# Gated linear attention before two mixtures of experts: the recurrence in chunks of 64 tokens in place of 128, and the last expert weighed in its hidden blocks

## The chip, the cores and the metric

The kernel is one program on one core of a Trainium2 chip. A core has five engines, each with its own queue of instructions: TensorE (PE in the rows, its weight loads PEld), VectorE (DVE), ScalarE (ACT), GpSimd (POOL) and SyncE (SP), which here only starts DMAs. They wait for each other through semaphores. PE multiplies a stationary block held in a 128x128 array by a moving block and writes to eight PSUM banks of 128 partitions by 512 floats. The metric is the device time of one execution in microseconds, median of several.

## The reference

For 4 sequences of 768 tokens and 8 heads with 48 channels, a gated recurrence gives `y`; two feed-forward stages follow on all 3072 tokens.

```
state = alpha[t, :, None] * state + k[t] (x) v[t]      # per head, 48 x 48
y[t]  = q[t] @ state
h = x @ w_in                       # 384 -> 2048
g = h if h > 0 else exp(h) - 1
x2 = g @ w_out                     # 2048 -> 384
p = domain_probs / (sum(domain_probs) + 1e-9)
out = sum over 4 experts e of p[:, e] * (relu(x2 @ w1[e]) @ w2[e])   # 384 -> 1024 -> 384
```

## The kernel before, in words

**The feed-forward work** runs in 6 tiles of 512 tokens. A tile has 48 steps: 16 of the first stage (ELU) and 8 for each of 4 experts (ReLU). In step J of a tile PE computes the hidden block of step J+2 into `ps_h` (`hidden`, 9 matmuls of 512 columns), and then adds the block of step J into three banks `ps_o` (`output`, 9 matmuls). The 9 are 3 blocks times 3 products: each operand is split in a high and a low fp32r part, and high x low, low x high and high x high are added (L568 to L570). ACT makes the high part and DVE the low part, of each weight block (L927, L744), of each hidden block (L953 or L958, then L761 or L765), of the input `x` and of `x2`. PE waits before `output(J)` for `g_ready`, and before `hidden(n)` for the bank of block n-2 and the weights. In the last step of the ELU stage (J = 15) there is no `hidden` ahead: PE does `output(15)` and then `first_experts`, which needs `x2`, split by ACT and DVE from the banks that `output(15)` has just filled.

**The attention** runs in 12 units of 256 tokens. Two are done ahead of the first tile (functions with "early" in the name). The other ten, u = 2 to 11, are cut in pieces and dealt out between the steps: table `PARTS_AT` gives a step at which each kind of work starts, and a unit's "piece" i comes i steps later. In PE's queue a piece stands between `hidden(J+2)` and `output(J)`; in step 15 it stands between `output(15)` and `first_experts`. Even units from u = 4 start in step 5 of a tile, odd ones in step 28; units 2 and 3 start in steps 15 and 28 of tile 0. DVE, ACT and POOL take the events of step J-1 in their step J.

A chunk of 128 tokens is halved again and again: level l couples right and left spans of 2^l tokens. Levels 0 to 3 are done on DVE and POOL in blocks of 16 tokens, whose scores go out to memory and come back as `pair_weights`. Levels 4, 5 and 6 are matmuls of q and k (L440), whose results ACT copies as rectangles into `pair_weights` (L876), while DVE and POOL carry the decays into q (L730) and k (L1083). Then PE transposes the keys (L495), forms the outer products of keys and values (`outer`, L513, 32 columns of the array, 48 moving columns), DVE adds them to a state that POOL has decayed (L739, L1095), and `attend` gives the outputs of each chunk: 28 matmuls of a 128x32 stationary tile by 128 moving columns (L537 from the state, L541 and L546 from `pair_weights`). Four such tiles, side by side in the array's columns, run at once. Heads go in pairs: one head's 48 channels in partitions 0 to 47, the other's in 64 to 111.

The pieces of a unit are: level 4 at i = 0, level 5 at 2, level 6 at 4, keys at 6, outer products at 8, outputs of both chunks at 10. They share three PSUM banks `ps_att` in turn. PE sees one fp32 matmul as two records; an fp32r matmul is one.

**The end.** After the last block DVE multiplies each of three banks by the last expert's weight into `part` (L791), POOL adds it to `acc` (L1103), and SP stores `acc` (L376). There are two `part` buffers.

Of the kernel before, what the change touches and what calls it, by code (L numbers as in the profile page):

```python
# [5 lines left out]
F32 = mybir.dt.float32  # L6
# [12 lines left out]
LEVELS = 7  # L19
# [6 lines left out]
UNIT = 2 * P  # L26
UNITS = TOKENS // UNIT
# [16 lines left out]
BANK_AT = {("L", LOW): 0, ("L", LOW + 1): 2, ("L", LOW + 2): 4, ("K", 0): 6, ("KV", 0): 8, ("Y", 0): 9}  # L44
NBANK = 11
# [58 lines left out]
for lag in range(LEVELS - 2):  # L104
    EARLY_ORDER += [(0, lag + 2), (1, lag)]
EARLY_ORDER += [(1, LEVELS - 2), (1, LEVELS - 1)]

# [11 lines left out]
COUNTS = {"low": LEVELS, "block": PARTS + 1, "piece": max(PIECES) + 2}  # L119
# [9 lines left out]
def is_elu(n):  # L129
    return n % STEPS < N1  # L130

# [12 lines left out]
def program(nc, q_d, k_d, a_d, v_d, qb_d, kb_d, ab_d, k0_d, v0_d, w_d, probs_d, eye_d, masks_d, sc_d, pn_d, out):  # L144
    ctx = ExitStack()
    with ctx:
# [15 lines left out]
        TD += [sbs(f"decay{1 << l}", 2, [P, PAIRS, UNIT >> l]) for l in range(1, LEVELS + 1)]  # L162
        VT = sbs("v_tok", 2, [P, 2, PAIRS, P])
        PW = sb("pair_weights", [P, 2, HEADS, P])
        KS = sbs("k_tok", 2, [P, PAIRS, P])
        ST = sbs("state", 3, [P, PAIRS, 2 * D])
# [12 lines left out]
        ex = sbs("elu_exp", 2, [P, TILE])  # L179
        gt = sbs("elu_out", 2, [P, TILE])  # L180
# [7 lines left out]
        v0 = part[1][0:1, 0:PAIRS * 2 * D].rearrange("p (a e) -> p a e", a=PAIRS)  # L188
        early_w = pb[:].rearrange("p e t -> p (e t)").rearrange("p (c a t) -> p c a t", c=2, a=HEADS)
        weights = [PW[:], early_w]  # L190
# [36 lines left out]
        p_step = sem("p_step")  # L227
# [22 lines left out]

        def y_bank(g):
# [4 lines left out]
        def queries(g):  # L256

            return chunk(QT, g)

        def pair_weights(g):  # L260
            return weights[g // 2 if g < EARLY else 0][:, g % 2]
# [32 lines left out]
        def rectangles(banks, w, l, sd):  # L294

            h = 1 << l
            dst = w.rearrange("p c (a s) t -> p s c a t", s=2)[:, sd]
            if l < LEVELS - 1:
                src = banks[sd][:, 0:2 * PAIRS * h].rearrange("p (c a t) -> p c a t", c=2, a=PAIRS)
                for m in range(HALF // h):  # L300
                    rows = slice(2 * m * h, (2 * m + 1) * h)
                    yield dst[rows, :, :, (2 * m + 1) * h:(2 * m + 2) * h], src[rows]
            else:
                src = banks[sd][:, 0:PAIRS * h].rearrange("p (c a t) -> p c a t", c=2, a=PAIRS // 2)
                for i in range(2):
                    yield dst[0:h, :, 2 * i:2 * i + 2, h:2 * h], src[h * i:h * (i + 1)]

        @block.sync
        def _(sp):
# [39 lines left out]
            def place_scores(u):  # L349
# [4 lines left out]
                for c in range(2):  # L354
                    for b in range(P // SUB):
                        rows = slice(SUB * b, SUB * (b + 1))
                        sp.dma_start(PW[rows, c, :, rows], sc_d[u].rearrange("(h b) (s t) -> b s h t", h=HEADS, t=SUB)[P // SUB * c + b]
                                     ).then_inc(pw_in, 16)
# [55 lines left out]
        def _(pe):  # L414
            def bank_free(u, i):
# [8 lines left out]
                elif i == BANK_AT["KV", 0]:  # L424
                    pe.wait_ge(st_ready, 2 * u + 3)
                else:
                    pe.wait_ge(xa_ready, 2 * u + i - BANK_AT["Y", 0] + 1 - EARLY)

            def level(banks, s, l):

                h = 1 << l
                for c in range(2):
                    if l < LEVELS - 1:
                        blocks_of = [(pr, m, 2 * m * h, (PAIRS * c + pr) * h) for pr in range(PAIRS) for m in range(HALF // h)]
                    else:
                        blocks_of = [(2 * i + b, 0, i * h, (PAIRS // 2 * c + b) * h) for b in range(PAIRS // 2) for i in range(2)]
                    for pr, m, row, col in blocks_of:
                        for sd in range(2):
                            r, first = slice(HALF * sd, HALF * (sd + 1)), P * c + 2 * m * h
                            last = nc.tensor.matmul(banks[sd][row:row + h, col:col + h], KL[s][r, pr, first:first + h],  # L440
                                                    QT[s][r, pr, first + h:first + 2 * h], start=True, stop=True)
# [11 lines left out]
            def early_pairs(u, l):  # L453
# [12 lines left out]
                if l == LEVELS - 1:  # L466
                    level(banks, u, l).then_inc(e_step[u], 1)
                    return
# [11 lines left out]
            def first_state():  # L480
                pe.wait_ge(first_in, 32)
                for pr in range(PAIRS):
                    last = nc.tensor.matmul(ps_l[1][1][0][:, pr * 2 * D:(pr + 1) * 2 * D], k0[:, pr, :], v0[:, pr, :], start=True, stop=True)
                last.then_inc(kv_done, 1)

            def transpose_k(g):
                if g < EARLY:
                    pe.wait_ge(e_k[g // 2], LEVELS)
                    pe.wait_ge(e_rect[g // 2], LEVELS - 1 - MASKED)
# [8 lines left out]

            def outer(u):
                if u < LEAD:  # L500
                    pe.wait_ge(e_rect[u], LEVELS - MASKED)
                else:
                    bank_free(u, BANK_AT["KV", 0])
                o, s = kv_bank(u), u % 2
                pe.wait_ge(v_in[s], 16 * (u // 2 + 1))
                for c in range(2):
                    pe.wait_ge(ks_ready, 2 * u + c + 1)
                    for pr in range(PAIRS):
                        col = (PAIRS * c + pr) * D
                        for i in range(P // COL):  # L510
                            rows = slice(COL * i, COL * (i + 1))
# [4 lines left out]
            def attend(g):  # L516
                s = g // 2 % 2
                if g < EARLY:
                    pe.wait_ge(e_near, g // 2 + 1)
                    pe.wait_ge(e_rect[g // 2], LEVELS - MASKED)  # L520
                    pe.wait_ge(e_q[g // 2], LEVELS)
                    pe.wait_ge(ks_ready, min(g + 1, EARLY - 1))
                else:
                    pe.wait_ge(pw_in, 16 * 2 * (P // SUB) * (g // 2 - LEAD + 1))
                    pe.wait_ge(rect, 2 * lev(g // 2, LEVELS - 1))
                    pe.wait_ge(q_up, lev(g // 2, LEVELS - 1))
                    bank_free(g // 2, BANK_AT["Y", 0] + g % 2)
                o = y_bank(g)
                pe.wait_ge(st_ready, g + 1)
                pe.wait_ge(v_in[s], 16 * (g // 4 + 1))  # L530
                v = VT[s][:, g % 2]
                for kt in range(KT):
                    dst = [o[COL * i:COL * (i + 1), kt * P:(kt + 1) * P] for i in range(P // COL)]
                    heads = [4 * kt + i if kt < KT - 1 else 2 * i for i in range(P // COL)]
                    for d, head in zip(dst, heads):
                        left = D - COL // 2 if kt == KT - 1 else head % 2 * 2 * COL
                        nc.tensor.matmul(d, ST[g % 3][:, head // 2, left:left + COL], queries(g)[:, head // 2, :], start=True, stop=False)  # L537
# [649 lines left out]
```

## Time and profile before

| | |
|---|---|
| median of 3 runs | 1324.49 us (1324.25 to 1326.15) |
| profiled execution, its own time | 1323.65 us |
| its span, first to last instruction | 1321.6 us |
| granted TensorE clock, mean | 0.999 |
| busy: PE, DVE, ACT, POOL | 98%, 64%, 46%, 41% |

The span is what the rows cover; 2.05 us of the execution's own time lie outside it. "Busy" of PE counts the time in which at least one matmul is under way, and a matmul's own time (0.39 us for 512 columns) overlaps the next: what one costs is the distance from start to start. In a timeline row the columns are the start in us from the span's beginning, the time until the last of the merged instructions ends, engine, line, operation, tiles, shapes and the number of instructions.

### The profile page before, as it was taken

The numbers are of one execution on the slowest core, as the hardware profiler recorded it, in microseconds if no ns is written. First come the engines' busy times: TensorE is split into PE (matmuls) and PEld (weight loads), VectorE is DVE, ScalarE is ACT, GpSimd is POOL, SyncE is SP. The second block draws the span as 40 slices with busy tenths as digits, with TensorE's granted clock in tenths as the row PEclk, the third lists the DMA queues.
The fourth block names the chain that finished last, engine by engine and source line by source line (L and its number), as shares of the span: only waits on it lengthen the run. The fifth ranks groups of instructions, "written<-read, shape, count | busy, mean of one in ns | idle before, by whom it ended". The sixth has DMA issues, their size and how long they took to land.

```text
span 1321.6 us, 26257 instructions
## 1 busy us (share of the span) xinstructions
PE 1299.6 (98%) x10472; PEld 1070.5 (81%) x10472; DVE 844.8 (64%) x1121; ACT 607.1 (46%) x1051; POOL 537.6 (41%) x457
## 2 busy tenths in 40 slices
PE   6899999999999999999999999999999999999998
PEld 6787888888888888888888888888888888888886
DVE  7786767765676765576776567666557645654443
ACT  3656343367434347534336733435653433653331
POOL 1671948611755831453851175682155311100012
PEclk9999999999999999999999999999999999999999
DMA  5545263255244236235335524423633233523330
GB/s 199 179 132 174 80 198 90 87 171 169 87 150 147 75 102 215 98 108 201 89 99 170 170 85 144 144 86 110 203 103 113 86 98 86 155 90 108 96 96 24
DMA packets 84028, 165.77 MB, mean 125 GB/s; under 512 B 30146, under 2 KB 31683, under 8 KB 83908
## 3 DMA queue, kind: packets, MB, share of 16 engines
q1 hardware_dynamic: 83616, 163.97, 40.0%
q8 instruction: 83, 1.36, 0.4%
q14 instruction: 37, 0.30, 0.1%
q10 hardware_dynamic: 292, 0.13, 0.0%
HBM read 157.99 MB, written 6.08 MB: 124 GB/s over the span
## 4 chain that ended last, share of the span: by engine, by line
PE 88%; issue 5%; DVE 4%; ACT 2%; POOL 1%; DMA 0%; POOLq 0%; ACTq 0%; DVEq 0%
PE ps_o L568 14%; PE ps_h L568 13%; PE ps_h L569 13%; PE ps_h L570 13%; PE ps_o L569 13%; PE ps_o L570 13%; PE ps_att L440 2%; DVE w_lo L744 1%; PE ps_att L537 1%; PE ps_att L513 1%; POOL acc L1103 1%; DVE elu_out L757 1%; PE ps_att L495 1%; PE ps_att L541 1%; PE ps_att L546 1%
## 5 line engine op out<-in xcount | busy, mean ns | idle before, releaser
L744 DVE TENSOR_TENSOR w_lo<-w_stage,w_hi 128x768 fp32r<-128x768 f32 x288 | 341.5, 1186 | 30.7 <-ACT w_hi L927 27.1
L958 ACT ACTIVATE g_hi<-ps_h 128x512 fp32r<-128x512 f32 x192 | 114.8, 598 | 499.9 <-PE ps_h L570 499.8
L568 PE MATMUL ps_o<-g_hi,w_lo 128*128 128x512 f32 x864 | 342.5, 396 | 0.6 <-DVE g_lo L761 0.6
L568 PE MATMUL ps_h<-x_hi,w_lo 128*128 128x512 f32 x864 | 337.8, 391 | 2.7 <-DVE x_lo L751 1.3
L569 PE MATMUL ps_o<-g_lo,w_hi 128*128 128x512 f32 x864 | 336.7, 390 | 0.0
L570 PE MATMUL ps_o<-g_hi,w_hi 128*128 128x512 f32 x864 | 336.7, 390 | 0.0
L569 PE MATMUL ps_h<-x_lo,w_hi 128*128 128x512 f32 x864 | 336.3, 389 | 0.0
L570 PE MATMUL ps_h<-x_hi,w_hi 128*128 128x512 f32 x864 | 336.3, 389 | 0.0
L765 DVE SCALAR_TENSOR_TENSOR g_lo<-ps_h,g_hi 128x512 fp32r<-128x512 f32 x192 | 132.3, 689 | 262.4 <-ACT g_hi L958 262.1
L927 ACT CAST w_hi<-w_stage 128x768 fp32r<-128x768 f32 x288 | 239.4, 832 | 13.7 <-DMA w_stage<-in_w 12.7
L275 POOL TENSOR_TENSOR products<-blocks 128x384 f32<-128x384 f32 x150 | 195.3, 1316 | 87.1 <-DVE scores L680 81.5
L1103 POOL TENSOR_TENSOR acc<-acc,part 128x512 f32<-128x512 f32 x54 | 77.1, 1456 | 315.3 <-DVE part L791 315.3
L568 PEld LDWEIGHTS ps_h<-x_hi,w_lo 128*128 128x128 f32 x864 | 162.1, 188 | 40.7 <-issue 4.2
L568 PEld LDWEIGHTS ps_o<-g_hi,w_lo 128*128 128x128 f32 x864 | 162.1, 188 | 36.5 <-issue 1.2
L570 PEld LDWEIGHTS ps_o<-g_hi,w_hi 128*128 128x128 f32 x864 | 162.2, 188 | 34.3
L570 PEld LDWEIGHTS ps_h<-x_hi,w_hi 128*128 128x128 f32 x864 | 162.2, 188 | 33.9
L569 PEld LDWEIGHTS ps_h<-x_lo,w_hi 128*128 128x128 f32 x864 | 162.2, 188 | 33.4
L569 PEld LDWEIGHTS ps_o<-g_lo,w_hi 128*128 128x128 f32 x864 | 162.3, 188 | 31.9
L1083 POOL TENSOR_TENSOR k_level<-k_level,decay 128x512 f32<-128x512 f32 x30 | 36.2, 1206 | 230.9 <-PE ps_att L440 230.9
L761 DVE TENSOR_TENSOR g_lo<-elu_out,g_hi 128x512 fp32r<-128x512 f32 x96 | 70.8, 739 | 61.1 <-ACT g_hi L953 61.1
L757 DVE SCALAR_TENSOR_TENSOR elu_out<-elu_exp,ps_h 128x512 f32<-128x512 f32 x96 | 65.8, 685 | 65.1 <-ACT elu_exp L947 65.1
L953 ACT CAST g_hi<-elu_out 128x512 fp32r<-128x512 f32 x96 | 59.6, 621 | 94.1 <-DVE elu_out L757 60.2
(100 smaller groups left out, 999.1 us busy)
## 6 DMA issues: line engine op xcount, KB each, us to landing
w_stage<-in_w SPq DMA_DIRECT2D x288, 384.0 KB, 3.1
k_level<-in_k SPq DMA_DIRECT2D x12, 512.0 KB, 5.6
q_low<-in_q SPq DMA_DIRECT2D x12, 512.0 KB, 6.4
alpha<-in_a SPq DMA_DIRECT2D x12, 512.0 KB, 4.1
v_tok<-in_v SPq DMA_DIRECT2D x12, 512.0 KB, 5.1
p_rows<-p_norm SPq DMA_DIRECT2D x6, 1024.0 KB, 9.0
out<-acc SPq DMA_DIRECT2D x18, 256.0 KB, 3.9
blocks<-in_q_blocks SPq DMA_DIRECT2D x10, 384.0 KB, 4.0
```

The lines of the kernel that those rows point to most:

```text
L275: return engine.tensor_tensor(dst, q[:, :, 1, i:i + 1, :].broadcast_to([P, pairs, h, D]), k[:, :, 0], ALU.mult)
L568: nc.tensor.matmul(dst, lhs[1], rhs[0], start=first, stop=False)
L569: nc.tensor.matmul(dst, lhs[0], rhs[1], start=False, stop=False)
L570: return nc.tensor.matmul(dst, lhs[0], rhs[0], start=False, stop=last)
L744: nc.vector.tensor_tensor(wl[n % WRING][:], stage[n % STAGE][:], wh[n % WRING][:].bitcast(F32), ALU.subtract).then_inc(w_low, 1)
L757: nc.vector.scalar_tensor_tensor(gt[n % 2][:], ex[n % 2][:], -1.0, ps_h[n % 2][:], ALU.add, ALU.max).then_inc(h_read, 1)
L761: nc.vector.tensor_tensor(gl[n % GS][:], gt[n % 2][:], gh[n % GS][:].bitcast(F32), ALU.subtract).then_inc(g_ready, 1)
L765: nc.vector.scalar_tensor_tensor(gl[n % GS][:], ps_h[n % 2][:], 0.0, gh[n % GS][:].bitcast(F32), ALU.max, ALU.subtract).then_inc(g_ready, 1)
L927: nc.scalar.copy(wh[n % WRING][:], stage[n % STAGE][:]).then_inc(w_hi, 1)
L953: nc.scalar.copy(gh[n % GS][:], gt[n % 2][:]).then_inc(g_hi, 1)
L958: nc.scalar.activation(gh[n % GS][:], ps_h[n % 2][:], ACT.Relu).then_inc(g_hi, 1)
L1103: nc.gpsimd.tensor_tensor(acc[:, m, :], acc[:, m, :], part[k % 2][:], ALU.add).then_inc(acc_added, 1)
```

## The change

In the ten later units the recurrence goes in spans of 64 tokens. Level 6 is gone (`LEVELS` 7 to 6). The outer products are made for each span of 64 tokens: the same number of matmuls, but with 64 rows, 64 columns of the array and 64 moving columns, into two banks, one for each side. There are four new states in a unit instead of two, in a layout of 64 columns in which the head pair lies on row halves. DVE makes each with four instructions that multiply, add and read PSUM at once; POOL's decay (L1095) is gone there. The outputs are 128 matmuls of a 64x32 stationary tile by 64 moving columns, in two pieces: 64 from `pair_weights` and 32 from the states at i = 9, and the other 32 from the states, with row halves exchanged, at i = 11. The early units keep chunks of 128; their states lie in `acc` and one array of pair weights in the ELU buffers, and the state tiles there are 64 instead of 48 columns wide in PSUM. Last, for the final 8 blocks of all (the last expert of the last tile), DVE multiplies the hidden block by the expert's weight before it is split, and the end is an addition of PSUM to `acc` on DVE alone.

```diff
-LEVELS = 7
+EARLY_LEVELS = 7
+LEVELS = 6
+SPANS = UNIT // HALF
-CLEARS = 5
+CLEARS = 6
-PIECES = {0: ("L", LOW), 2: ("L", LOW + 1), 4: ("L", LOW + 2), 6: ("K", 0), 8: ("KV", 0), 10: ("Y", 0)}
-NBANK = 11
+PIECES = {0: ("L", LOW), 2: ("L", LOW + 1), 4: ("K", 0), 6: ("KV", 0), 9: ("Y", 0), 11: ("Y", 1)}
+NBANK = 10
+STATES_AT = {6: (0,), 7: (1, 2), 8: (3,)}
+X_AT = {11: 0, 12: 1}
...
+def is_weighed(n):
+    return n >= ALL - NE
...
-                    nc.tensor.matmul(ps_l[1][1][0][:, pr * 2 * D:(pr + 1) * 2 * D], k0[:, pr, :], v0[:, pr, :], start=True, stop=True)
+                    nc.tensor.matmul(ps_l[1][1][0][:, pr * P:(pr + 1) * P], k0[:, pr, :], v0[:, pr, :], start=True, stop=True)
...
             def outer(u):
...
-                            v = VT[s][:, c, pr, i // 2 * HALF:i // 2 * HALF + D]
-                            last = nc.tensor.matmul(o[rows, col:col + D], KS[c][:, pr, rows], v, start=True, stop=True)
+                        for i in range(2):
+                            for side in range(2):
+                                r, rows = slice(HALF * side, HALF * (side + 1)), slice(HALF * i, HALF * (i + 1))
+                                last = nc.tensor.matmul(kv_banks(u)[side][rows, col:col + HALF], KS[c][r, pr, rows], VT[s][r, c, pr, rows],
+                                                        start=True, stop=True)
...
+            def state_part(u, turn):
+                for c in range(2):
+                    for wide in range(2):
+                        for pr in range(PAIRS):
+                            for span in range(2):
+                                sd = span ^ turn
+                                r, first, left = slice(HALF * sd, HALF * (sd + 1)), P * c + HALF * span, COL * (sd ^ wide)
+                                last = nc.tensor.matmul(y_part(u, c, span, KT - 1 if wide else sd, pr),
+                                                        ST[(SPANS * (u - LEAD) + 2 * c + span) % STATES][r, pr, left:left + COL],
+                                                        QT[u % 2][r, pr, first:first + HALF], start=False, stop=(turn == c == wide == 1))
+                return last
+
+            def value_part(u):
+                for c in range(2):
+                    for sd in range(2):
+                        for wide in range(2):
+                            for pr in range(PAIRS):
+                                for span in range(2):
+                                    r, left = slice(HALF * span, HALF * (span + 1)), HALF * sd + COL * (sd ^ wide)
+                                    nc.tensor.matmul(y_part(u, c, span, KT - 1 if wide else sd, pr), VT[u % 2][r, c, pr, left:left + COL],
+                                                     PW[r, c, 2 * pr + sd, :], start=(c == sd == wide == 0), stop=False)
+
+            def attend(u):
...
+                value_part(u)
+                pe.wait_ge(st_ready, states_before(u, SPANS - 1))
+                state_part(u, 0).then_inc(y_done, 1)
+
+            def attend_other(u):
+                pe.wait_ge(y_done, 2 * u + 1)
+                state_part(u, 1).then_inc(y_done, 1)
...
+            def state(u, k):
...
+                for pr in range(PAIRS):
+                    col = (PAIRS * (k // 2) + pr) * HALF
+                    last = nc.vector.scalar_tensor_tensor(ST[(g + 1) % STATES][:, pr, :], ST[g % STATES][:, pr, :], TD[LEVELS][u % 2][:, pr, k:k + 1],
+                                                          kv_banks(u)[k % 2][:, col:col + HALF], ALU.mult, ALU.add)
...
+            def weigh_hidden(n):
+                dve.wait_ge(h_full, n + 1)
+                nc.vector.scalar_tensor_tensor(gt[n % 2][:], ps_h[n % 2][:], 0.0, pb[:, EXPERTS - 1, :], ALU.max, ALU.mult).then_inc(weighed, 1)
+                lower_elu(n)
+
+            def add_last(t):
...
+                    nc.vector.tensor_tensor(acc[:, m, :], ps_o[m][:], acc[:, m, :], ALU.add).then_inc(acc_added, 1)
...
-            weigh(TILES - 1, EXPERTS - 1)
+            add_last(TILES - 1)
```

How instructions move, at two places. First PE's queue in tile 1, around steps 14 to 16, where the outputs of unit 4 stand. Before, in step 15, after the last product of `output(15)` and ahead of `first_experts`:

```order
L570 MATMUL ps_o<-g_hi,w_hi 128x512
L537 MATMUL ps_att<-q_low,state 32x128 x4
L541 MATMUL ps_att<-pair_weights,v_tok 32x128 x4
L537 MATMUL ps_att<-q_low,state 32x128 x4
L541 MATMUL ps_att<-pair_weights,v_tok 32x128 x4
L537 MATMUL ps_att<-q_low,state 32x128 x4
L546 MATMUL ps_att<-pair_weights,v_tok 32x128 x8
...
L568 MATMUL ps_h<-x_hi,w_lo 128x512
```

(the middle six rows come once more, for the second chunk). Now, in step 14 between `output(13)` and `output(14)`, and the rest in step 16 between `hidden(18)` and `output(16)`:

```order
L659 MATMUL ps_o<-g_hi,w_hi 128x512
L616 MATMUL ps_att<-pair_weights,v_tok 32x64 x64
L602 MATMUL ps_att<-q_low,state 32x64 x32
L657 MATMUL ps_o<-g_hi,w_lo 128x512
...
L659 MATMUL ps_h<-x_hi,w_hi 128x512
L602 MATMUL ps_att<-q_low,state 32x64 x32
L657 MATMUL ps_o<-g_hi,w_lo 128x512
```

The 56 matmuls have become 96 and 32, and no piece stands in step 15 of tiles 1 to 4 any more.

Second, DVE's queue where an odd unit's states are made, among weight splits (`w_lo`) and hidden splits (`g_lo`). Before (L739 is the addition to the state):

```order
L739 TENSOR_TENSOR state<-ps_att,state 64x4x48 [waits state_decayed,kv_done]
L739 TENSOR_TENSOR state<-ps_att,state 64x4x48
L680 TENSOR_REDUCE scores<-products 128x2x4 [waits product] x2
L744 TENSOR_TENSOR w_lo<-w_stage,w_hi 128x768 [waits w_hi_ready]
L765 SCALAR_TENSOR_TENSOR g_lo<-ps_h,g_hi 128x512 [waits g_hi_ready]
```

Now, in the step with two states:

```order
L840 SCALAR_TENSOR_TENSOR state<-state,decay_1,ps_att 128x64 [waits decay_ready,y_done,kv_done,state_ready]
L840 SCALAR_TENSOR_TENSOR state<-state,decay_1,ps_att 128x64 x3
L840 SCALAR_TENSOR_TENSOR state<-state,decay_1,ps_att 128x64 [waits decay_ready,y_done,kv_done,state_ready]
L840 SCALAR_TENSOR_TENSOR state<-state,decay_1,ps_att 128x64 x3
L758 TENSOR_TENSOR q_low<-q_low,decay_0 128x128x4 [waits decay_ready,q_low_updated]
L846 TENSOR_TENSOR w_lo<-w_stage,w_hi 128x768 [waits w_hi_ready]
L866 SCALAR_TENSOR_TENSOR g_lo<-ps_h,g_hi 128x512 [waits g_hi_ready]
```

Eight short instructions stand ahead of the splits in that step, and four in the step before and in the one after it; before there were two in each of two steps.

## Rows read from the trace of the kernel before

**Rows 1.** The profile's page: PE's busy time, and the chain that ended last.
```profile
PE 1299.6 (98%) x10472; PEld 1070.5 (81%) x10472; DVE 844.8 (64%) x1121; ACT 607.1 (46%) x1051; POOL 537.6 (41%) x457
PE 88%; issue 5%; DVE 4%; ACT 2%; POOL 1%; DMA 0%; POOLq 0%; ACTq 0%; DVEq 0%
```
**Rows 2.** PE's waits: line, who ended them, us in total, times, longest.
```profile
PE ps_o L483 <- DMA part<-in_v_first: 4.5, 1, 4.5
PE ps_h L568 <- DVE x_lo L751: 1.3, 1, 1.3
```
**Rows 3.** Timeline of PE, tile 1, around level 5: eight matmuls, piece, nine matmuls.
```profile
299.80 0.39 PE L568 MATMUL ps_h<-x_hi,w_lo 128*128 128x512 f32 x1
...
301.61 0.39 PE L570 MATMUL ps_h<-x_hi,w_hi 128*128 128x512 f32 x1
301.93 0.76 PE L440 MATMUL ps_att<-q_low,k_level 64*32 64x32 f32 x64
...
304.81 0.39 PE L568 MATMUL ps_h<-x_hi,w_lo 128*128 128x512 f32 x1
```
**Rows 4.** The same around level 4.
```profile
292.05 0.39 PE L570 MATMUL ps_h<-x_hi,w_hi 128*128 128x512 f32 x1
292.37 1.22 PE L440 MATMUL ps_att<-q_low,k_level 64*16 64x16 f32 x128
...
295.71 0.39 PE L568 MATMUL ps_h<-x_hi,w_lo 128*128 128x512 f32 x1
```
**Rows 5.** The same around level 6.
```profile
310.70 0.39 PE L570 MATMUL ps_h<-x_hi,w_hi 128*128 128x512 f32 x1
311.02 0.69 PE L440 MATMUL ps_att<-q_low,k_level 64*64 64x64 f32 x32
...
313.82 0.39 PE L568 MATMUL ps_h<-x_hi,w_lo 128*128 128x512 f32 x1
```
**Rows 6.** The same around the outer products.
```profile
328.78 0.39 PE L570 MATMUL ps_h<-x_hi,w_hi 128*128 128x512 f32 x1
329.10 0.89 PE L513 MATMUL ps_att<-v_tok,k_tok 128*32 128x48 f32 x64
...
332.08 0.39 PE L568 MATMUL ps_o<-g_hi,w_lo 128*128 128x512 f32 x1
```
**Rows 7.** The same around the outputs of unit 5 (112 records in between).
```profile
440.76 0.39 PE L570 MATMUL ps_h<-x_hi,w_hi 128*128 128x512 f32 x1
...
446.47 0.40 PE L568 MATMUL ps_h<-x_hi,w_lo 128*128 128x512 f32 x1
```
**Rows 8.** Timeline, tile 5, steps 14 to 15, where no attention is left.
```profile
1181.26 0.69 DVE L761 TENSOR_TENSOR g_lo<-elu_out,g_hi 128x512 fp32r<-128x512 f32 x1 [0.69 <-ACT g_hi L953]
1182.47 0.39 PE L568 MATMUL ps_o<-g_hi,w_lo 128*128 128x512 f32 x1
1184.28 0.39 PE L570 MATMUL ps_o<-g_hi,w_hi 128*128 128x512 f32 x1
1184.86 0.47 PE L568 MATMUL ps_h<-x_hi,w_lo 128*128 128x512 f32 x1 [0.19 <-DVE x_lo L771]
```
**Rows 9.** Timeline of the end: PE's last matmul, POOL's and DVE's last work.
```profile
1315.62 0.39 PE L570 MATMUL ps_o<-g_hi,w_hi 128*128 128x512 f32 x1
1315.46 3.71 POOL L1103 TENSOR_TENSOR acc<-acc,part 128x512 f32<-128x512 f32 x3 [23.49 <-DVE part L791]
1316.84 0.69 DVE L791 TENSOR_TENSOR part<-ps_o,p_rows 128x512 f32<-128x512 f32 x1 [0.78 <-POOL acc L1103]
```
**Rows 10.** Groups by line: busy us, mean ns of one, idle before.
```profile
L739 DVE TENSOR_TENSOR state<-ps_att,state 64x192 f32<-64x192 f32 x48 | 16.8, 351 | 0.9 <-PE ps_att L513 0.5
L765 DVE SCALAR_TENSOR_TENSOR g_lo<-ps_h,g_hi 128x512 fp32r<-128x512 f32 x192 | 132.3, 689 | 262.4 <-ACT g_hi L958 262.1
L797 DVE TENSOR_SCALAR p_sum<-p_sum 128x24 f32<-128x24 f32 x1 | 0.6, 644 | 0.0
```
**Rows 11.** Timeline of DVE before step 0.
```profile
54.62 0.69 DVE L757 SCALAR_TENSOR_TENSOR elu_out<-elu_exp,ps_h 128x512 f32<-128x512 f32 x1
```

More of the change, by code:

```diff
@@ L118, with states_before @@
 }
-COUNTS = {"low": LEVELS, "block": PARTS + 1, "piece": max(PIECES) + 2}
+COUNTS = {"low": LEVELS, "block": PARTS + 1, "piece": max(X_AT) + 1}
+def states_before(u, k):
+    return EARLY + 1 + SPANS * (u - LEAD) + k
 def segment(n):
@@ L249, in kv_bank, with kv_banks @@
             return ps_l[0][u][1 - u] if u < LEAD else bank_of("KV", u, 0)
+        def kv_banks(u):
+            return [bank_of("KV", u, side) for side in range(2)]
         def y_bank(g):
@@ L497, in transpose_k, with early_outer @@
                 last.then_inc(kt_done, 1)
-            def outer(u):
[L500 to L504, printed above, removed]
+            def early_outer(u):
+                pe.wait_ge(e_rect[u], EARLY_LEVELS - MASKED)
+                o = kv_bank(u)
+                pe.wait_ge(v_in[u], 16)
+                for c in range(2):
+                    pe.wait_ge(ks_ready, 2 * u + c + 1)
+                    for pr in range(PAIRS):
+                        col = (PAIRS * c + pr) * HALF
+                        for i in range(P // COL):
+                            rows = slice(COL * i, COL * (i + 1))
+                            v = VT[u][:, c, pr, i // 2 * HALF:(i // 2 + 1) * HALF]
+                            last = nc.tensor.matmul(o[rows, col:col + HALF], KS[c][:, pr, rows], v, start=True, stop=True)
+                    last.then_inc(kv_done, 1)
+            def outer(u):
+                s = u % 2
+                for side in range(2):
+                    bank_free(u, BANK_AT["KV", 0] + side)
                 pe.wait_ge(v_in[s], 16 * (u // 2 + 1))
@@ L548, in attend @@
-                last.then_inc(y_done, 1)
+                    dst = [o[COL * i:COL * (i + 1), kt * P:(kt + 1) * P] for i in range(PAIRS)]
+                    left = (0, HALF, COL)[kt]
+                    for pr, d in enumerate(dst):
+                        nc.tensor.matmul(d, early_st[g % 3][:, pr, left:left + COL], q[:, pr, :], start=True, stop=False)
+                    sides = (0, 1) if kt == KT - 1 else (kt,)
+                    for sd in sides:
+                        left = HALF * sd + COL * ((kt == KT - 1) != (sd == 1))
+                        for pr, d in enumerate(dst):
+                            last = nc.tensor.matmul(d, v[:, pr, left:left + COL], w[:, 2 * pr + sd, :], start=False, stop=(sd == sides[-1]))
@@ L562, in attention @@
                     outer(u)
-                else:
-                    for c in range(2):
-                        attend(2 * u + c)
+                elif l == 0:
+                    attend(u)
+                else:
+                    attend_other(u)
             def products(dst, lhs, rhs, first, last):
```

319 lines of the change are left out of this document (167 added, 152 removed).

## The prediction

> **What bounds the kernel now.** I read the page first: PE is busy 98% of the span, and the chain of work that ended last is PE for 88% [rows 1]. Then the list of PE's waits: apart from 4.5 us for the first DMA, the largest at the hidden blocks is 1.3 us, once [rows 2]. So PE's queue is full from the first hidden block to the last output, and the time is what PE's instructions cost from start to start, plus a head of about 50 us and a tail. Third, the timeline of PE around each kind of piece. Eight steps from one 512-column matmul to the next take 301.61 - 299.80 = 1.81 us, so 0.2265 us each [rows 3]. 5184 of them are 1174 us; that part is untouched. Between the last product of a hidden block and the first of the next lie ten such steps, 2.27 us; with a piece in between, what is above 2.27 is the whole price of the piece:
> level 4: 3.66 - 2.27 = 1.39 [rows 4]; level 5: 3.20 - 2.27 = 0.93 [rows 3]; level 6: 3.12 - 2.27 = 0.85 [rows 5]; outer products: 3.30 - 2.27 = 1.03 (nine matmuls and the step over the piece, again ten) [rows 6]; outputs: 5.71 - 2.27 = 3.44 [rows 7].
>
> **How these prices are made.** An fp32 matmul is two records. In level 6, 32 records in 0.69 us, of which the last alone is about 0.22: 0.47 us for 8 groups of four tiles, 59 ns a group [rows 5]. [...] Level 4 does not follow this: 128 records in 1.22 - 0.17 us are 8.2 ns a record, however few its columns are (16); that is the pace at which records can be started [rows 4]. What is left of each price is fixed, the change of tile shape and back: 0.85 - 0.47 = 0.38 in level 6, 1.03 - 0.68 = 0.35 in the outer products, 1.39 - 1.05 = 0.34 in level 4, and 3.44 - 28 x 0.109 = 0.39 in the outputs. I take 0.38.
>
> **The change, part by part, for each of the ten later units.**
> Level 6 goes: -0.85. With it go an update of q on DVE and of k on POOL and four copies on ACT; none of these held PE, so they count nothing.
> Outer products: 64 records in 16 groups of 2x2 tiles with 64 columns, the shape of level 6: 16 x 0.059 + 0.38 = 1.32, +0.29.
> Outputs: 128 matmuls are 256 records, in two pieces. Eight tiles (64x32) can be under way together. A group of eight would need 59 ns by columns, but 8 x 8.2 = 66 ns by the pace of starting, so the second decides: 192 x 0.0082 + 0.38 = 1.95, and 64 x 0.0082 + 0.38 = 0.90. Together 2.85, -0.59. No row shows eight tiles with so many columns at once. From below the price is 32 groups x 0.059 + 0.76 = 2.65; from above, if only four tiles run at a time, 64 x 0.059 + 0.76 = 4.54. I take 2.85, since rows 5 and 6 show both halves of the arrangement, and level 4, which uses the same eight places, kept its 8.2 ns.
> [...]
> Sum for a unit -0.85 + 0.29 - 0.59 = -1.15, for ten -11.5 us.
>
> **Step 15 of tiles 1 to 4.** Before, the outputs of the even unit stood between `output(15)` and the first expert and covered the splitting of x2 by ACT and DVE. Now nothing stands there. Tile 5 has no piece in that place either and shows the price: 1184.86 - 1184.28 = 0.58 instead of 0.23, and the first block after it is a little slow [rows 8]. 0.4 us, four times: +1.6. Below it is 0 (nothing else can gain), above perhaps 1.0 each if DVE comes late.
> Would it? In tile 5 the last split of block 15 ends at 1181.95, and `output(15)` starts at 1182.47: 0.5 us to spare [rows 8]. The new kernel puts eight state instructions ahead of it on DVE in step 13, but also 1.95 us of output piece on PE in step 14: 2.45 to spare. The size of a state instruction (128x64, reading PSUM): 192 columns take 351 ns, 512 take 689 [rows 10], so 1.06 ns a column and 148 fixed, 216 ns for 64 columns; eight are 1.7 us. Before there was nothing of this kind in that step. Part of it fills time in which DVE waited for ACT: it idles 262 us before the 192 splits of L765 alone [rows 10]. I cost it at nothing. The upper bound is the slowest small instruction with a scalar operand, 644 ns for 24 columns [rows 10]: eight would be 5.2 us, 2.7 past what is to spare, and PE would then wait some 1 to 2 us in each of four tiles, +6. Odd units stand in the ReLU stage, where PE runs 3 blocks (6 us) between a hidden block and the next use of its bank: nothing even then. Queued behind the states on DVE are one weight split and one hidden split, and PE waits for both two steps later.
> Other new waits: `attend_other` waits for PE's own earlier piece, over 5 us back; the outputs wait for the third state, made a step before. POOL has less to do, SP's queue is as before.
>
> **The early units.** Two outer products go from 48 to 64 moving columns in groups of 1x4: 16 x 13.3 ns = 0.21 each, both on PE's path. The additions to a state take 64 more columns, 0.07 for each of two halves, and stand in the path two or three times; one of them is in DVE's row up to the first ELU at 54.62, which ends the wait before step 0 [rows 2, 11]. Together +0.7 (0.3 to 1.2). The larger first matmul should be free: its weight load of 128 columns is as long.
>
> **The end.** PE's last matmul ends at 1316.01. Before, DVE's last product waited for a buffer that POOL held (start 1316.84), and POOL ended at 1315.46 + 3.71 = 1319.17 [rows 9]. Now DVE adds the last bank right away: 1316.05 + 0.69 = 1316.75. -2.4 us; the three stores come closer together, which may take back a few tenths. The weighed blocks cost DVE and ACT more (689 becomes about 690 + 740 on DVE), in 8 steps of about 4.1 us in which DVE then does 2.6 us; a hidden block has 6 us until it is missed, its chain takes about 2.4. Nothing.
>
> **Sum.** -11.5 + 1.6 + 0.7 - 2.4 = -11.6 us. From the profiled execution's own 1323.65 us that makes 1312.0; the median, 1324.49, stands 0.84 above, so 1312.9.
>
> **Rivals.**
> A, slower: the array takes only four of the eight output tiles at once. For it: no row has eight with 64 columns. Against it: level 6 reads two row halves at once and fills two banks, the outputs before fill four column groups at once, and the new form moves no more data at a time than these two do together. Then outputs cost 4.54 instead of 3.44, a unit +0.54, the sum +5.4 - 0.1 = +5.3: 1329.8. It decides as soon as a record takes over 12 to 13 ns in place of 8.2. Chance 7%.
> B, the gain halves: records start no faster than they did in the outer products, 0.68 / 64 = 10.6 ns. Outputs are then 256 x 0.0106 + 0.76 = 3.47, a unit -0.53, the sum -5.4: 1319.1. [...] Chance 6%.
> C: DVE's states cost two or three times 216 ns and PE waits in the ELU stage: +3 to +6, 1317. Chance 6%.
> [...]
> [...]
>
> **How the numbers follow.** Forecast 79%, A 7, B 6, C 6, D 2. The forecast alone spans 1309.5 (outputs at their lower bound, -2; early units free) to 1316 (starting pace 5% worse, step 15 at 0.8, stores late). The range reaches to C and stops short of B: 1309.5 to 1318. What a measurement can tell from no change is 0.2%, 2.65 us, so faster means below 1321.8: the forecast, B, C, 90% with a margin for what I haven't seen; slower is A and a little, 7%; the same 3%.
>
> **What would show it.** In the new profile: PE still at 98%; the two output pieces with 192 and 64 records over about 1.6 and 0.55 us; the outer products over 0.97 us; no level with 64-column tiles in the later units; a wait of 0.2 to 0.4 us after `output(15)` in four tiles; state instructions of about 0.22 us; the last addition on DVE ending 0.7 us after PE. It would be wrong if a record in the output pieces took over 10 ns, if the fixed 0.38 grew for the 64x32 form, or if PE waited for DVE in step 15 by more than a microsecond.

## The result and the profile after

The changed kernel takes 1335.1 us (median of five, 1332.3 to 1337.5) against 1324.5 before: ratio 1.0075, 95% interval 1.0064 to 1.0086. It is slower by 10.6 us where 11.6 us faster were forecast. The profiled execution took 1332.47 us by its own time, span 1330.7.

The page and the list of PE's waits come first, as in [rows 1, 2]:
```profile
PE 1301.6 (98%) x11592; PEld 1069.4 (80%) x11592; DVE 851.2 (64%) x1239; ACT 595.4 (45%) x1011; POOL 499.2 (38%) x415
q8 instruction: 92, 1.51, 0.5%
```
```profile
PE ps_att L602 <- issue: 9.0, 5, 2.0
PE ps_o L525 <- DMA part<-in_v_first: 4.5, 1, 4.5
PE ps_h L658 <- issue: 1.3, 1, 1.3
PE ps_h L657 <- DVE x_lo L852: 1.3, 1, 1.3
```
The share of busy time is the same 98%, so it hides the loss. The list of waits shows it: five waits, 9.0 us together, in front of a state matmul of the outputs (L602), and one of 1.3 us in front of a product. "issue" says that the profile shows no semaphore, buffer or other engine that ended them. I call such a pause in the middle of PE's work a hole. Before, no such wait existed among the later units.

Each of the five lies inside the first output piece, here in that of unit 2 (timeline of PE):
```profile
162.95 0.39 PE L659 MATMUL ps_h<-x_hi,w_hi 128*128 128x512 f32 x1
163.27 1.43 PE L616 MATMUL ps_att<-pair_weights,v_tok 64*32 64x64 f32 x124
...
164.56 0.71 PE L602 MATMUL ps_att<-q_low,state 64*32 64x64 f32 x47
167.28 0.34 PE L602 MATMUL ps_att<-q_low,state 64*32 64x64 f32 x13 [2.01 <-issue]
```
Record for record the piece stands still in the middle of a loop, 13 records before its end. The DMA view of just this stretch (163.27 to 167.28, 40 slices of 0.1 us) shows what moved then:
```profile
DMA  0000000000000070000000000000000000055929
q8 instruction: 1, 0.02, 1.9%
```
Up to the 35th slice one packet is all that moves: 16 KB on the instruction queue, put in the slice in which it starts, from 164.67. Its 1.9% of 16 engines' 4.01 us are 1.2 us, so it ends at 165.9, and the matmuls go on 1.4 us later, at 167.28. The five pieces without such a hole run through (unit 11; the last row is the tenth step, as in [rows 7]), and so do the second piece, the outer products and level 5:
```profile
1088.37 0.39 PE L659 MATMUL ps_h<-x_hi,w_hi 128*128 128x512 f32 x1
1088.69 1.43 PE L616 MATMUL ps_att<-pair_weights,v_tok 64*32 64x64 f32 x124
...
1092.90 0.39 PE L657 MATMUL ps_h<-x_hi,w_lo 128*128 128x512 f32 x1
...
1098.79 0.39 PE L659 MATMUL ps_h<-x_hi,w_hi 128*128 128x512 f32 x1
1099.11 0.86 PE L602 MATMUL ps_att<-q_low,state 64*32 64x64 f32 x64
...
1102.10 0.40 PE L657 MATMUL ps_h<-x_hi,w_lo 128*128 128x512 f32 x1
```
```profile
1074.81 0.39 PE L659 MATMUL ps_h<-x_hi,w_hi 128*128 128x512 f32 x1
1075.13 1.16 PE L568 MATMUL ps_att<-v_tok,k_tok 64*64 64x64 f32 x64
...
1078.40 0.39 PE L657 MATMUL ps_h<-x_hi,w_lo 128*128 128x512 f32 x1
```
Less the ten steps of 2.27 us these are 2.26, 1.04 and 1.32 us. With the 0.85 of level 6 gone, these rows make a unit 0.70 cheaper than before; the median piece of each kind over all units, unrounded and with levels 4 and 5 each 0.01 lower, makes it 0.74, which the books below use. 1.15 were forecast. The transposition of k costs what it did.

A hole has a second price. After two of the five, PE's granted clock falls from 1.00 to 0.50 for some 3 us (windows: time, busy time of each engine with its count, then PEclk):
```profile
767.50:770.50 3.00, 1.23 (x70) 0.97 (x57) 2.31 (x7) 1.35 (x2) 2.92 (x4) 0.97 0.46 139
770.50:773.60 3.10, 3.10 (x9) 2.33 (x9) 0.41 (x1) 0.00 (x0) 3.10 (x4) 0.50 0.39 127
773.60:776.60 3.00, 2.81 (x13) 2.04 (x11) 1.15 (x2) 1.64 (x3) 2.86 (x4) 0.98 0.00 0
```
Nine records fit into the second stretch, thirteen into the third; seven products take 0.43 us instead of 0.23 each time, 1.5 us. PE's busy time in the first stretch is 1.23 of 3.00 us: the hole comes first, the clock follows.

What was forecast elsewhere came. Step 15 of tile 1, eight states on DVE, and the end, where DVE adds the last bank straight after PE, as against [rows 8, 9]:
```profile
345.39 0.39 PE L659 MATMUL ps_o<-g_hi,w_hi 128*128 128x512 f32 x1
345.97 0.47 PE L657 MATMUL ps_h<-x_hi,w_lo 128*128 128x512 f32 x1 [0.19 <-DVE x_lo L886]
```
```profile
336.64 1.74 DVE L840 SCALAR_TENSOR_TENSOR state<-state,decay,ps_att 128x64 f32<-128x64 f32 x8
```
```profile
1326.16 2.05 DVE L881 TENSOR_TENSOR acc<-ps_o,acc 128x512 f32<-128x512 f32 x3 [2.69 <-PE ps_o L659]
1327.09 0.39 PE L659 MATMUL ps_o<-g_hi,w_hi 128*128 128x512 f32 x1
```
The books for the profiled executions, in us: pieces -7.4; holes in the outputs +10.0 (the gap between two records, 1.8 to 2.2 each); the hole behind a level-4 piece at 301.9 +1.4; half clock +3; first product 1.8 later; step 15 +1.4; the tail after PE's last product 3.2 instead of 5.6, -2.4. Sum +7.8; the profiled executions differ by 8.8.

### The profile page after: what moved, and what is told of

Read it like the earlier page. It is cut to its first block, busy times and chain, and to the rows that moved or that the text cites. A ratio compares the mean times of both kernels' runs of the same rounds, so it can differ in the third digit from the quotient of the medians.

```text
span 1330.7 us, 28490 instructions
## 1 busy us (share of the span) xinstructions
PE 1301.6 (98%) x11592; PEld 1069.4 (80%) x11592; DVE 851.2 (64%) x1239; ACT 595.4 (45%) x1011; POOL 499.2 (38%) x415
## 4 chain that ended last, share of the span: by engine, by line
PE 91%; DVE 5%; issue 2%; ACT 2%; DMA 0%; ACTq 0%; DVEq 0%
PE ps_o L657 15%; PE ps_h L657 14%; PE ps_o L659 14%; PE ps_o L658 14%; PE ps_h L658 14%; PE ps_h L659 14%; PE ps_att L471 1%; PE ps_att L602 1%; DVE w_lo L846 1%; PE ps_att L616 1%; PE ps_att L568 1%; DVE elu L858 1%; PE ps_att L537 1%; ACT g_hi L1069 1%; DVE g_lo L862 1%
## 5 line engine op out<-in xcount | busy, mean ns | idle before, releaser
L846 DVE TENSOR_TENSOR w_lo<-w_stage,w_hi 128x768 fp32r<-128x768 f32 x288 | 330.4, 1149 | 27.4 <-ACT w_hi L1043 24.1
L1074 ACT ACTIVATE g_hi<-ps_h 128x512 fp32r<-128x512 f32 x184 | 110.1, 598 | 484.0 <-PE ps_h L659 484.0
L866 DVE SCALAR_TENSOR_TENSOR g_lo<-ps_h,g_hi 128x512 fp32r<-128x512 f32 x184 | 126.9, 690 | 266.0 <-ACT g_hi L1074 266.0
L306 POOL TENSOR_TENSOR products<-blocks 128x384 f32<-128x384 f32 x150 | 200.7, 1353 | 180.6 <-DVE scores L768 133.0
L1220 POOL TENSOR_TENSOR acc<-acc,part 128x512 f32<-128x512 f32 x51 | 73.4, 1469 | 336.9 <-DVE part L906 336.9
L862 DVE TENSOR_TENSOR g_lo<-elu,g_hi 128x512 fp32r<-128x512 f32 x104 | 80.6, 776 | 66.6 <-ACT g_hi L1069 61.1
L858 DVE SCALAR_TENSOR_TENSOR elu<-elu,ps_h 128x512 f32<-128x512 f32 x96 | 65.8, 686 | 63.5 <-ACT elu L1063 63.5
L1069 ACT CAST g_hi<-elu 128x512 fp32r<-128x512 f32 x96 | 59.6, 621 | 99.4 <-DVE elu L858 65.5
L1203 POOL TENSOR_TENSOR k_level<-k_level,decay 128x512 f32<-128x512 f32 x20 | 23.0, 1152 | 202.3 <-PE ps_att L471 202.3
```

The source lines that it names most:

```text
L306: return engine.tensor_tensor(dst, q[:, :, 1, i:i + 1, :].broadcast_to([P, pairs, h, D]), k[:, :, 0], ALU.mult)
L846: nc.vector.tensor_tensor(wl[n % WRING][:], stage[n % STAGE][:], wh[n % WRING][:].bitcast(F32), ALU.subtract).then_inc(w_low, 1)
L858: nc.vector.scalar_tensor_tensor(gt[n % 2][:], ex[n % 2][:], -1.0, ps_h[n % 2][:], ALU.add, ALU.max).then_inc(h_read, 1)
L862: nc.vector.tensor_tensor(gl[n % GS][:], gt[n % 2][:], gh[n % GS][:].bitcast(F32), ALU.subtract).then_inc(g_ready, 1)
L866: nc.vector.scalar_tensor_tensor(gl[n % GS][:], ps_h[n % 2][:], 0.0, gh[n % GS][:].bitcast(F32), ALU.max, ALU.subtract).then_inc(g_ready, 1)
L1069: nc.scalar.copy(gh[n % GS][:], gt[n % 2][:]).then_inc(g_hi, 1)
```

## The experiments

**The theory (F).** The page gives PE 11592 matmul and 11592 weight-load records and the instruction queue 92 packets of 16.4 KB; before 10472, 10472 and 83:
```profile
q8 instruction: 83, 1.36, 0.4%
```
With PE's semaphore waits (456 and 496 instructions) that is 257 and 258 instructions a packet. A packet is 16384 bytes, 63.8 for each of the 257. So PE's program arrives in blocks of 256 instructions of 64 bytes. In the changed kernel the 1280 fp32 matmuls of the outputs are 2560 matmul records (L602 and L616) and 2560 weight loads, the 5184 fp32r products 5184 and 5184: an fp32 matmul is four instructions and a product two. The first output piece is 384 instructions in 1.9 us. A border is the place where one block ends and the next begins. Counted through the program, all five holes stand at one place, 193 or 194 modulo 256, which is a border of blocks, and always the *second* border inside the piece. Where the first border lies 62, 65, 103, 105 or 108 instructions after the piece's start (units 5, 10, 2, 3, 8) there is a hole; at 19, 151, 189, 194 and 232 there is none. From 151 on the second border is behind the piece, among products of 0.23 us. So a block is fetched while the one before it runs, and the fetch takes longer (3.5 us in unit 2, from the first border at 163.79 to the first matmul after the hole) than 256 small instructions do (1.3 us).

The packets' own times in the traces close the chain. In all 20 holes inside output pieces, in this kernel and in three of those below, the last packet before PE goes on starts 0.1 to 2.4 us (in 18 of them 0.7 to 1.4) after the border ahead of the hole's, takes 0.9 to 1.7 us, and PE goes on 1.2 to 1.6 us after the packet has ended, wherever in the piece that is.

**Rivals.** W: the holes are a wait for DVE's states, inside the piece. T: the output tiles simply disturb each other; the holes are a matter of the piece, at random.

**The outputs in three pieces.**
```
- 9: ("Y", 0), 11: ("Y", 1)      # 64 value + 32 state matmuls; 32 state matmuls
+ 9: ("Y", 0), 10: ("Y", 1), 11: ("Y", 2)      # 64 value; 32 state; 32 state
```


> Theory F (instruction supply): in the changed kernel TensorE issues the first piece of outputs, 384 instructions, in 1.9 us, and five of the ten pieces contain a hole of 1.8 to 2.2 us because the piece reaches a second border between blocks of 256 instructions while the fetch of that block is still under way. Here the same instructions stand in pieces of 256, 128 and 128 at steps 14, 15 and 16: no hole over 1 us in any output piece, so 10.0 us less, and no half granted clock behind the holes (3.3 us less). Step 15 is covered again (its wait of 0.35 us in four tiles goes: -1.4), one more piece per unit costs 0.4 (+4). Forecast 1321.5 us, 1319 to 1324. Rival W (the holes are the states' wait inside the piece, on VectorE's states): they stand at step 14 or 15 as before, in the same units, and the time stays at 1331 to 1336. Rival T (the output tiles simply run slower side by side, the holes being lost records): the time stays within 2 us of the changed kernel's.

Measured 1320.05 us (1319.3 to 1320.8), ratio to before 0.9965 (0.9953 to 0.9978). No output piece has a hole, no stretch of products runs at half clock, step 15 has no wait. The waits that are left, and unit 3, which had a hole of 1.9 us:
```profile
PE ps_o L525 <- DMA part<-in_v_first: 4.6, 1, 4.6
PE ps_h L518 <- DVE k_level L789: 1.6, 1, 1.6
PE ps_att L518 <- DVE k_level L789: 1.6, 1, 1.6
PE ps_h L662 <- issue: 1.3, 1, 1.3
```
```profile
223.11 0.39 PE L663 MATMUL ps_h<-x_hi,w_hi 128*128 128x512 f32 x1
223.43 1.48 PE L616 MATMUL ps_att<-pair_weights,v_tok 64*32 64x64 f32 x128
224.84 0.50 PE L661 MATMUL ps_o<-g_hi,w_lo 128*128 128x512 f32 x1
...
229.16 0.86 PE L602 MATMUL ps_att<-q_low,state 64*32 64x64 f32 x64
```
The same instructions, with those of the states moved between other products, take 15 us less. The wait of 1.3 us that is left is the hole behind the level-4 piece of unit 4, at the same instruction as in the changed kernel. T falls. W does not by this run alone, since the states are now read a step later; the shift below decides on it.

**All outputs in one piece.**
```
- 9: ("Y", 0), 11: ("Y", 1)
+ 9: ("Y", 0)                    # attend(u); attend_other(u)
```


> All 128 output matmuls of a unit (512 instructions) in one piece at step 14. Theory F: the piece spans at least two block borders in every unit, and at the alignment of this program nine of the ten pieces (all but the sixth, unit 7) reach the second border before its block is there: nine holes of 1.6 to 2.2 us instead of five, +7 us, against 0.4 us less per unit for the piece that is gone (-4) and step 15's longer wait where a tile's second unit would have ended (0 to +1); half clock behind some of them (up to +1.6 each). Forecast 1337, 1333 to 1343. Rival W (states' wait): the number of holes stays five in the same units, 1328 to 1331. Rival T: 1328 to 1331.

Measured 1345.0 us (1343.6 to 1348.2), ratio 1.0156. PE's list of waits:
```profile
PE ps_att L602 <- issue: 18.8, 9, 3.4
```
Nine holes, and the piece without one is that of unit 7 (no gap over 0.32 us). The places are as forecast; the time is 2 us above the range. Against the changed kernel's profiled execution it is +15.7: holes +9.8; six stretches at half clock with 45 products instead of two with 14, +6.2; the wait for PE's own first half, which now stands inside the piece (`y_done`, 0.27 us, found below), +2.7; one piece less per unit -3.8; sum +14.9. One of the six, after unit 3's hole, as windows:
```profile
226.60:231.80 5.20, 3.34 (x248) 2.66 (x249) 4.00 (x5) 1.32 (x2) 5.04 (x5) 1.00 0.33 86
231.80:235.90 4.10, 4.10 (x41) 3.22 (x31) 0.00 (x0) 0.00 (x0) 0.62 (x1) 0.58 0.25 90
```

**The same program, its borders moved by 128 instructions.**
```
+ if J < 8:
+     for _ in range(32):
+         pe.wait_ge(eye_in, 16)     # long full; two waits share an instruction
```


> The changed kernel with 128 more semaphore-wait instructions on TensorE, 16 on each of eight of its first steps, all on a semaphore that is full long before: they move every later block border by 128 instructions against the pieces and do nothing else. Theory F: the holes stand in other units: in units 4, 9 and 11 (border 66, 104 and 61 instructions after the start of the piece, where the five with holes now have 61 to 108) and no longer in units 2, 3, 5, 8 and 10: three holes instead of five, -4 us, less some half clock, + the price of 128 waits (0 to 3 us; the instructions are taken while the matmuls before them run). Forecast 1329, 1325 to 1334; the places decide, not the time. Rivals W and T: holes stay in units 2, 3, 5, 8 and 10, the time does not fall.

The page counts 128 instructions more than for the changed kernel (28618, 28490): the 256 waits of the source are 128 instructions.

Measured 1326.6 us (1324.7 to 1329.3), ratio 1.0015. Four holes, in units 4, 6, 9 and 11: the three forecast and one at 23 instructions, which I had taken for safe because 19 was. Units 2, 3, 5, 8 and 10 have none. Unit 4, which ran through in the changed kernel:
```profile
PE ps_att L602 <- issue: 7.7, 4, 2.0
```
```profile
333.02 0.51 PE L602 MATMUL ps_att<-q_low,state 64*32 64x64 f32 x29
335.41 0.46 PE L602 MATMUL ps_att<-q_low,state 64*32 64x64 f32 x31 [1.88 <-issue]
```
Instructions that compute nothing, some 250 us ahead, decide which piece stands still. W falls too: the wait for the states stands once in a piece, after 256 of its instructions, and the holes of these kernels stand 22 to 108 instructions behind it, in the midst of the states' matmuls, and have moved with the borders. The hole behind unit 4's level-4 piece is gone too, but a pause of 0.5 us stands inside unit 7's level-4 piece, which has 256 instructions and a border just ahead of its first and another at its 250th.

That first hole shows what else counts. It stands at the same border in the changed kernel, in three pieces, in one piece and in the two versions of two pieces below, and costs 1.4, 1.4, 0.9, 0.5 and 0 us beyond a product's step; the packet started 2.3, 2.5, 1.9, 1.8 and 0.7 us after the border before. What delays a packet no run shows.

**The last expert's part alone, on the kernel before.**
```
+ weigh_hidden(n), high_weighed(n) in the last 8 hidden blocks; add_last(TILES - 1)
- add_part(TILES - 1, EXPERTS - 1)
```


> The kernel before with the last expert's part of the change alone (its weights multiplied into its hidden blocks of the last tile on VectorE, the four accumulators read straight at the end). As forecast for this part: the end after the last big matmul goes from 5.6 to 3.2 us, -2.4: 1322.1 us, 1321.3 to 1323.0. Rival: the adding of the last tile was not what the end stood on, or the weighing holds up TensorE in the last expert's steps: 1324 to 1326.

Measured 1321.8 us (1321.4 to 1322.7), ratio 0.9979 (0.9970 to 0.9988): -2.9 against a forecast of -2.4. This part is right and independent of the rest.

**The price of the waits: the kernel before with the same 128.**

> The kernel before with the same 128 waits in its first eight steps as the shifted changed kernel: the price of the waits alone. Its largest piece is 256 instructions in 1.05 us, so Theory F expects no hole in any piece at any alignment but a marginal one, and the waits hidden behind the matmuls before them: 1324.7 us, 1324 to 1326.5. If the waits cost more, the shifted and the aligned kernel have to be corrected by it; if holes of about 2 us appear in its pieces, the border matters already at 256 instructions.

Measured 1325.2 us, ratio 1.0009 (0.9999 to 1.0019): 0 to 2.5 us, no hole in any piece of the later units. The kernel before had no piece of over 256 instructions in a rush.

**Borders placed by hand, pieces of 384 kept.**
```
+ PADS = 44 waits on steps 0-7, 44 or 40 on steps 112-119, 28 on steps 210-215
```


> The changed kernel with its pieces as they are (384 instructions at step 14), and 432 semaphore-wait instructions more on TensorE, all on a full semaphore: 176 in its first eight steps, 172 between the pieces of units 6 and 7, 84 before that of unit 11. They put the first block border of each output piece at 10 to 18 or at 140 to 231 instructions after its start, where none of the 30 such pieces seen so far had a hole (holes stood at 23 and at 61 to 108). Theory F: no hole in any of the ten output pieces (a short one, under 1 us, can be in unit 9, whose second border falls just behind the piece), no half clock: the changed kernel's 1335 less 10.0 of holes, less 1.4 (level-4 hole moved away), less 3 of half clock, + the price of the waits (0 to 4 us): 1321.5, 1318.5 to 1325. Rival (the holes belong to pieces of 384 instructions as such, about half of them at random): four to six holes, 1330 or more.

Measured 1325.7 us (1322.6 to 1327.6), ratio 1.0004; above the range. In its profile:
```profile
PE ps_att L603 <- issue: 2.6, 2, 1.6
PE ps_o L658 <- DVE g_lo L870: 2.2, 1, 2.2
```
Eight pieces have no hole, among them all seven with the border at 140 or more. The two holes stand where the border is 18 and 16 instructions in (gaps of 1.2 and 1.8 us); at 13 there is none. So the line that I had put at 19 runs through 13 to 20, and holes near it can be shorter. The packets tell why: where there is no hole, at 19 and 13, the packet had started 2.4 and 1.5 us *before* PE came to the first border, so the request ran ahead of PE; at 18 and 16 it started 0.1 and 0.7 us after it. What makes the request run ahead in one piece and not in the next is not shown. Behind two of the eight pieces without a hole (units 5 and 9, border at 142 and 140) the second border comes among products, and one came 0.3 and 0.6 us late. The third wait is another thing: DVE did two weight splits before a hidden split in step 16 of unit 6 and PE waited 2.2 us for it, after which the clock was half for seven products. It was seen in this one profile; whether the padding caused it was not tried. The rival "at random" is out all the same: of 30 pieces of 384 instructions in three kernels, all nine with the border at 23 to 108 have a hole, two of four at 13 to 19, and none of 17 at 140 or more.

**The outputs in two pieces of 256.**
```
- 9: ("Y", 0), 11: ("Y", 1)
+ 9: ("Y", 0), 10: ("Y", 1)      # 64 value; wait for the states, 32 state, y_done, 32 state
```


> The outputs of a unit in two pieces of 256 instructions each, the values (64 matmuls) at step 14 and both halves of the states (64 matmuls) at step 15; otherwise the changed kernel. Theory F: a piece of 256 instructions holds two block borders only where the first stands at its very first instructions, so no output piece has a hole; against the kernel of three pieces one piece fewer per unit, 10 x 0.38 = -3.8: 1316.2 us, 1315 to 1318. Rival (a piece's fixed cost is not what the third piece costs, or the states are not ready a step earlier than in three pieces, where the second half stood at step 16): 1319 to 1322. Rival (pieces of 256 have holes too, when they follow each other one step apart): holes of about 2 us at step 14 or 15, 1322 or more.

The median of five executions is 1319.4 us, but one of them, the profiled one, took 4.5 ms and says nothing; the other four (1318.3 to 1319.8) have a median of 1319.0. That is 2.8 us above the forecast of 1316.2, so it was run again:

> The kernel with the outputs in two pieces of 256 instructions once more, since the profiled execution of its first job was a disturbed one (4.5 ms) and says nothing, while its four others gave 1318.3 to 1319.8 us against a forecast of 1316.2. The time is expected at 1319 again. What is open is where the 2.8 us went: holes of 1 to 2 us in or behind a piece (Theory F would then need them at a border that stands at the first 20 instructions of a piece of 256, in units 4 and 7), a wait for the states or a bank at step 15, or a piece of 64 matmuls that costs more than two of 32 less a fixed cost (1.64 expected, 2.06 before).

Measured 1319.6 us (1318.2 to 1320.5), ratio 0.9957 (0.9944 to 0.9969), no hole in an output piece. The piece of states, as a timeline row, is
```profile
443.71 1.77 PE L602 MATMUL ps_att<-q_low,state 64*32 64x64 f32 x128
```
against two of 0.86 in the kernel of three pieces. The price over the products is 1.93 us instead of 2 x 1.03. Between the halves the records show a gap of 0.27 us: `pe.wait_ge(y_done, 2u+1)`, PE's wait for its own first half to be written, which costs nothing when the halves are steps apart. So a piece fewer saves 0.12 us and not 0.38: 2.6 us of the 2.8 that were missing (3.4 by this run's median).

> The same two pieces, but the states at step 16, a step later, as the changed kernel has its second piece. If the states or a bank hold up the piece at step 15, this one is faster or equal but for the wait at step 15 that it leaves uncovered (1.4 us in all): 1318 or less. If not, it is slower by those 1.4 us and by more holes or none: 1320 to 1321.

Measured 1320.3 us, ratio 0.9966 (0.9952 to 0.9979): the states don't hold up step 15; a step later only leaves it uncovered.

The versions of two and of three pieces beat both kernels, by 0.43% (0.31 to 0.56) and 0.35% against before. Their intervals overlap.

## Why the prediction was wrong, point by point

**PE stays full: wrong, and the step that failed.** "So PE's queue is full from the first hidden block to the last output, and the time is what PE's instructions cost from start to start ..." That held before, where the largest piece was 256 instructions in 1.05 us and no piece of the later units had a hole. I priced the output piece at the pace of starting records and put 192 of them into one piece, but did not ask what supplies PE at 4 to 5 ns an instruction. The page shows the queue (83 packets of 16 KB); it was not read. Price: 10.0 us of holes, 1.4 behind a level-4 piece (which met an unlucky border and a late packet; it was no larger than before), and 3 us of half clock: 14.4 of the 22 us between forecast and result (2.7 of it lie between the profiled execution and the median, which no profile shows). Shown by the three pieces, the one piece and the shift.

**Outputs at 8.2 ns a record: size off, the mechanism right in part.** Measured 2.26 for 1.95 and 1.04 for 0.90, 0.45 a unit, 4.5 us. The rows of the three-piece kernel give (1.48 - 0.86) / 64 = 9.7 ns a record. Record by record, the second and the third eight come in 56 ns each, and later ones mostly in about 67 ns, which is the 8.2 of level 4, with slower stretches of up to 162 ns in between. Those I had not priced; what makes them was not tried. And 8.2 ns is not the fastest pace "at which records can be started": 56 ns for eight are 7.0. Rival A (four tiles at a time) is excluded by the 56 ns, D (a unit costs what it did) by the 0.70 us that a unit is cheaper; B's 10.6 ns was nearer to the truth than mine, which the chances of 79 to 6 did not say.

**The old prices under it.** The 0.68 us of the outer products is (0.89 - 0.21) of rows 6, 42.5 ns for a group of four. The 0.109 for the outputs is in the trace of before: in unit 5 (L537, L541, L546) the records start in fours, 6 to 7 ns apart, and 109 ns from four to four. At the products' 226.5 ns for 512 columns [rows 3] twice the moving columns is 42.5 ns for 48, 56.6 for 64 and 113 for 128, beside 42.5, 59 and 109 measured.

**Fixed cost 0.38 a piece:** held: 2.26, 1.04 and, for the third piece, 1.03 us, less 9.7 ns a record, leave 0.40, 0.42 and 0.41. That it is the change of tile shape was my reading; no run shows what it is made of. It does not hold where a piece contains its own wait.

**Level 6 gone, outer products +0.29:** right (1.32 measured, 1.32 forecast).

**Step 15 +0.4 in four tiles:** right (0.58 for 0.23, four times). **DVE's states free:** right: eight take 1.74 us (1.7 forecast), no wait of PE in step 13 to 16 comes from them; rival C did not come.

**The early units +0.7:** the first product starts 1.8 us later in the changed kernel, 0.8 later in three pieces, 1.9 in the second run of two. It scatters by a microsecond. The 0.21 us for each of two pieces of outer products is right where the granted clock is 1.00: a group of four takes 55.9 ns in the second of them (L552, from 45.6 us) and 42.7 before (L513), 16 x 13.3 ns = 0.21 us. The first (from 38.3 us) takes 107 ns a group in the changed kernel, 16 x 51 ns or 0.8 us more, but 56 in three pieces. In the kernel of one piece it takes 107 too, and there the granted clock is 0.50 (36 to 39 us); the changed kernel's trace has no clock record before 39.8 us. The larger first matmul was free: 0.214 us from start to start for 0.213. No cause is shown for the rest.

**The end -2.4:** right, -2.9 by itself.

**The range.** Its lower end, 1309.5, doesn't follow from its own terms: 1312.9 - 2 - 0.7 is 1310.2. Nothing hangs on it here.

Had there been no holes, the same pieces would have given -7.4 + 1.4 + 1.8 - 2.4 = -6.6 by this profile, 1318, at the edge of the range. The chance of 7% for slower stood on one mechanism of the array; that an engine could run out of *instructions* was among no rival.

## What to carry to other kernels

Look at how many instructions an engine takes per microsecond, not only at what each costs: here TensorE stood still in 11 of the 13 pieces of 384 instructions in which it went from one border of 256 instructions to the next in 1.3 us of work. Output pieces of small fp32 matmuls (four instructions each) ran through as long as they had 256 instructions at most, with long matmuls around them; but two level-4 pieces of 256 cost 0.5 and 1.4 us, so that size is no guarantee. "issue" waits in the middle of a loop, always at the same count of instructions modulo 256, are the sign; adding idle instructions ahead moves them, and a packet of the instruction queue that ends shortly before PE goes on confirms them. When a bound says "the engine is full", ask which resource of that engine the change loads that nothing loaded before, and keep a rival for it.

## What the runs showed of the hardware that was not expected

- PE's instructions come in blocks of 256 (16.4 KB a packet, 92 packets, 1.2 us each by their 0.5% of 16 engines' span). After a hole PE went on 1.2 to 1.6 us after the packet's end. Nine pieces with the first border 23 to 108 instructions in had gaps of 1.8 to 2.25 us; in the piece of 512 up to 3.6.
- After 9 of 20 holes (2 of 5 in the changed kernel, 6 of 9 in one piece, 1 of 4 with the shift, none of 2 in the aligned one) and after the wait for DVE in the last, PE's products came at 0.43 instead of 0.23 us, six to nine of them; where windows were read, the granted clock there was 0.50. Before it PE had stood still for some 2 us; which hole does it, the profiles do not tell.
- Eight 64x32 tiles with 64 moving columns do run together: 56 ns for eight fp32 records early in a piece, where four tiles took 59 ns in [rows 5] and 64 columns of a product take 28 (226.5 ns for 512).
